# Router logits of the last two pairs from eight more value columns, and two transfers moved behind the value products

## What is computed

```python
def _attn_ref(q, k, v):                      # per batch and head
    scores = scale * np.matmul(q, k.transpose(0, 1, 3, 2))
    kth = np.partition(scores, -top_k, axis=-1)[..., -top_k:-top_k + 1]
    scores = np.where(scores >= kth, scores, -1000000000.0)
    attn = softmax(scores)
    return np.matmul(attn, v)

x = attn_out.transpose(0, 2, 1, 3).reshape(B * S, H * D)   # 1152 x 512
logits = x @ w_gate                          # 512 x 8
expert_idx = np.argmax(logits, axis=1)       # gate_w: its softmax value
# token i takes the next free place (of 288) of its expert, in token order
h = np.maximum(disp[e] @ w1[e], 0.0)         # 512 -> 1024
y = h @ w2[e]                                # 1024 -> 512
out[i] = gate_w[i] * y[expert_idx[i], pos[i]]
```

## Time and profile before

| | us |
|---|---|
| median of 3 runs | 462.11 |
| lowest and highest run | 460.56, 462.35 |
| the profiled execution | 461.55 |
| its span in the trace | 459.8 |

### The profile page before, as it was taken

One profiled execution on the slowest core, in us unless ns is written; L12 is line 12 of the kernel. 1 busy time (PEld: TensorE's weight loads), 2 busy tenths in 40 slices (PEclk: granted clock), 3 DMA queues, 4 the chain that ended last, 5 costly groups with the idle time before them and its releaser, 6 DMA issues.

```text
span 459.8 us, 8667 instructions
## 1 busy us (share of the span) xinstructions
PE 404.1 (88%) x2753; PEld 343.3 (75%) x2753; DVE 288.6 (63%) x1405; ACT 237.8 (52%) x420; POOL 231.7 (50%) x223
## 2 busy tenths in 40 slices
PE   2986768989898898895889998999999999999993
PEld 1553336778686776784779897987999999999771
DVE  2699999899999999989999965401012212121210
ACT  2233358988887887867688992132212121222320
POOL 4044479789888898897799814032001010120310
PEclk9999956999999999999898999999999999999997
DMA  4220132023050230321100105978999685867500
GB/s 103 54 51 3 42 102 52 3 65 107 17 155 1 58 114 1 119 94 70 26 2 2 27 3 163 365 264 259 357 339 339 237 283 185 272 230 247 180 22 19
DMA packets 53633, 57.84 MB, mean 126 GB/s; under 512 B 34382, under 2 KB 34382, under 8 KB 53584
## 3 DMA queue, kind: packets, MB, share of 16 engines
q1 hardware_dynamic: 51408, 52.51, 36.3%
q0 software_dynamic: 2176, 4.73, 2.8%
HBM read 45.39 MB, written 13.92 MB: 129 GB/s over the span
## 4 chain that ended last, share of the span: by engine, by line
PE 35%; POOL 4%; issue 3%; DMA 3%; ACT 2%; DVE 2%; SPq 1%; DVEq 0%; POOLq 0%; ACTq 0%
PE ps_s L865 12%; PE ps_s L883 11%; PE ps_o L665 4%; PE ps_o L840 3%; PE ps_t L637 3%; DMA scores<-dispatched 2%; POOL probs L485 2%; POOL rest L480 1%; ACT pT L972 1%; PE ps_s L691 1%; PE ps_o L821 1%; PE ps_t L809 1%; DMA dispatched<-x,r_slot 1%; ACT probs L954 1%; SPq L405 1%
## 5 line engine op out<-in xcount | busy, mean ns | idle before, releaser
L480 POOL TENSOR_TENSOR rest<-below,scores 128x576 f32<-128x576 f32 x69 | 96.1, 1409 | 47.4 <-DVE below L1137 47.4
L665 PE MATMUL ps_o<-v_aug,pT 128*128 128x128 f32 (+2 forms) x800 | 102.8, 278 | 1.0 <-ACT pT L972 1.0
L665 PEld LDWEIGHTS ps_o<-v_aug,pT 128*128 128x128 f32 (+1 forms) x800 | 96.0, 185 | 2.9 <-issue 1.6
L485 POOL TENSOR_TENSOR probs<-scores,probs 128x576 f32<-128x576 f32 x66 | 93.3, 1431 | 0.7 <-ACT probs L948 0.6
L1072 DVE MAX8 cand<-scores 128x8 f32<-128x96 f32 x432 | 72.7, 257 | 12.1 <-ACT scores L922 12.1
L1038 ACT ACTIVATE scores<-ps_s 128x288 f32<-128x288 f32 x64 | 25.9, 411 | 103.8 <-PE ps_s L865 100.9
L637 PE MATMUL ps_t<-ident,probs 128*128 128x128 f32 (+1 forms) x360 | 55.8, 288 | 21.3 <-ACT pT L972 15.4
L865 PE MATMUL ps_s<-scores 128*128 128x192 f32 (+3 forms) x448 | 66.5, 306 | 0.0
L637 PEld LDWEIGHTS ps_t<-ident,probs 128*128 128x128 f32 (+1 forms) x360 | 38.1, 139 | 36.6 <-issue 21.7
L865 PEld LDWEIGHTS ps_s<-scores 128*128 128x128 f32 x448 | 64.4, 191 | 1.0 <-issue 0.7
L922 ACT ACTIVATE scores<-ps_s 128x576 f32<-128x576 f32 x72 | 46.0, 646 | 36.2 <-PE ps_s L607 20.4
(11 more groups left out here) (138 smaller groups left out, 405.4 us busy)
## 6 DMA issues: line engine op xcount, KB each, us to landing
w_sb<-in_moe_w_dram SPq DMA_DIRECT2D x9, 2048.0 KB, 12.8
scores<-in_moe_w_dram SPq DMA_DIRECT2D x7, 2048.0 KB, 10.9
dispatched<-empty SPq DMA_DIRECT2D x18, 257.0 KB, 3.6
scores<-dispatched SPq DMA_DIRECT2D x21, 192.8 KB
out_dram<-empty SPq DMA_DIRECT2D x9, 256.0 KB, 3.0
q_nat<-in_q_dram SPq DMA_DIRECT2D x16, 128.0 KB, 2.3
k_nat<-in_k_dram SPq DMA_DIRECT2D x16, 128.0 KB, 2.4
v_aug<-in_v_dram SPq DMA_DIRECT2D x16, 128.0 KB, 2.4
```

The costliest lines, as they stand in the source:

```text
L480: nc.gpsimd.tensor_tensor(rest[:, n % 3, :], below[:, n % 3, :], score_tile(n), ALU.mult).then_inc(rest_ready, 1)
L485: nc.gpsimd.tensor_tensor(probs[:, n % PROBS, :], score_tile(n), probs[:, n % PROBS, :], ALU.subtract).then_inc(masked_ready, 1)
L665: last = nc.tensor.matmul(dst, lhs, v_aug[:, g % 2, c, h, 0:width], start=(c == 0), stop=(c == TT - 1))
```

## The change

**Votes instead of logits for pairs 6 and 7.** The product of a head's output with its rows of the gate weights equals the attention applied to (values times gate weights). The change computes that small matrix, 8 columns per head, once per pair and early: SyncE loads the values of pairs 6 and 7 a second time, into the columns of `x` that these pairs will fill later (`values_of`), and the gate weights once more, laid out per head (`wg_heads`). At steps 10 to 13 TensorE transposes them (`turn_values`), ScalarE copies (`copy_vT`), TensorE multiplies (`vote`), and ScalarE keeps the result (`keep_votes`). `place_votes` writes it behind the column of ones in `v_aug` before pair 6 and before pair 7. The value products then give 73 columns per head instead of 65, and `normalise` divides the eight new ones into `voted`. The transposes of `x` for blocks 6 and 7, their copies and their logits are gone. The last head of `x` is scaled (`scale_head`) after the experts of batch 1 are chosen.

**Two transfers later.** SyncE waits for the last value product before it loads the second expert's first weights, and GpSimd waits for it before batch 0's scatter.

The core of the diff:

```diff
-    TURNED = {TILES * 2: 0, TILES * 3: 1, TILES * 4: 2, TILES * 5: 3, TILES * 6 - 2: 4, TILES * 6 + FULL: 5, TILES * 7 + FULL: 6}
-    SPARE = FULL * (D + 1) + P
+    TURNED = {TILES * 2: 0, TILES * 3: 1, TILES * 4: 2, TILES * 5: 3, TILES * 6 - 2: 4, TILES * 6 + FULL: 5}
+    VOTED = PAIRS - 2
+    VOTE_AT = TILES + 1
+    VOTES_AT = {TILES * (VOTED - 1) + 5: 0, TILES * VOTED + 5: 1}
+    WIDE = D + 1 + E
+    SPARE = FULL * WIDE + P
...
+            sp.wait_ge(wg_clean, 1)
+            for h in range(2):
+                sp.dma_start(wg_heads[h * D:(h + 1) * D, :, h, :],
+                             w_gate.rearrange("(c h d) e -> h d c e", h=2, d=D)[h][:, CH - 2:CH]).then_inc(wg_heads_loaded, 16)
+            for i in range(2):
+                load_heads(VOTED + i, v_h, values_of(i).rearrange("p t (h d) -> p t h d", h=2), v_nat_loaded[i])
...
-            sp.wait_ge(masked_ready, 2 * HELD)
+            sp.wait_ge(pv_done, ALL)
             load_w1(1, second)
...
             def scatter_tokens(b):
                 pool.wait_ge(drams_filled, 16 * (E * CAP // P + N // P))
                 pool.wait_ge(slots_ready, b + 1)
+                pool.wait_ge(pv_done, ALL)
+                pool.wait_ge(x_ready, 2 * PAIRS_PER_B * (b + 1))
                 for t in range(TT):
...
             def load_and_transpose(g, transposed):
+                if g == 2:
+                    pe.wait_ge(votes_kept, 4)
 
                 pe.wait_ge(qk_loaded, LOADS * (g + 1))
...
+                    if g >= VOTED:
+                        pe.wait_ge(votes_placed, 2 * (g - VOTED + 1))
...
-                            width = D + 1 if h == 1 and r == FULL - 1 else P
-                            dst = ps_o[:, h, r * (D + 1):r * (D + 1) + width]
+                            width = WIDE if h == 1 and r == FULL - 1 else P
+                            dst = ps_o[:, h, r * WIDE:r * WIDE + width]
...
+            def turn_values(i, naturals):
+
+                pe.wait_ge(v_nat_loaded[i], VLOADS)
+                pe.wait_ge(nat_copied, 2 * naturals)
+                if i > 0:
+                    pe.wait_ge(votes_kept, 2 * i)
+                for t in range(TT):
+                    rows = P if t < FULL else TAIL
+                    last = nc.tensor.transpose(ps_t[:, t * P:t * P + rows], values_of(i)[0:rows, t, :], ident[0:rows, 0:rows])
+                last.then_inc(vT_in_psum, 1)
+
+            def vote(i):
+
+                pe.wait_ge(vT_copied, i + 1)
+                pe.wait_ge(wg_heads_loaded, 32)
+                for t in range(TT):
+                    rows = P if t < FULL else TAIL
+                    last = nc.tensor.matmul(VOTE[0:rows, t * 2 * E:(t + 1) * 2 * E], xT[:, i, t * P:t * P + rows],
+                                            wg_heads[:, i].rearrange("p h e -> p (h e)"), start=True, stop=True)
+                last.then_inc(votes_in_psum, 1)
...
+                if VOTE_AT <= s < VOTE_AT + 4:
+                    if (s - VOTE_AT) % 2 == 0:
+                        turn_values((s - VOTE_AT) // 2, naturals)
+                    else:
+                        vote((s - VOTE_AT) // 2)
...
             pe.wait_ge(hot_placed, TT)
-            place_first_batch(0, 4)
-            transpose_x(2 * CH - 1, ALL)
-            place_first_batch(4, 7)
-            logits(2 * CH - 1)
+            place_first_batch(0, 10)
             carry_ranks()
-            place_first_batch(7, 13)
             router_ranks(1)
-            place_first_batch(13, CH * TT)
+            place_first_batch(10, CH * TT)
+            pe.wait_ge(x_ready, 2 * PAIRS)
...
+            def copy_vT(i):
+                act.wait_ge(vT_in_psum, i + 1)
+                nc.scalar.activation(xT[:, i, 0:S], ps_t[:, 0:S], ACT.Copy).then_inc(vT_copied, 1)
+
+            def keep_votes(i):
+                act.wait_ge(votes_in_psum, i + 1)
+                nc.scalar.activation(votes[:, i, 0:FULL], VOTE[:, 0:FULL * 2 * E].rearrange("p (t h e) -> p t h e", t=FULL, h=2),
+                                     ACT.Copy).then_inc(votes_kept, 1)
+                nc.scalar.activation(votes[0:TAIL, i, FULL], VOTE[0:TAIL, FULL * 2 * E:].rearrange("p (h e) -> p h e", h=2),
+                                     ACT.Copy).then_inc(votes_kept, 1)
+
+            def place_votes(i):
+                g = VOTED + i
+                act.wait_ge(votes_kept, 4)
+                act.wait_ge(pv_done, TILES * (g - 1))
+                nc.scalar.activation(v_aug[:, g % 2, 0:FULL, :, D + 1:WIDE], votes[:, i, 0:FULL], ACT.Copy).then_inc(votes_placed, 1)
+                nc.scalar.activation(v_aug[0:TAIL, g % 2, FULL, :, D + 1:WIDE], votes[0:TAIL, i, FULL],
+                                     ACT.Copy).then_inc(votes_placed, 1)
...
+                if VOTE_AT <= s < VOTE_AT + 4:
+                    if (s - VOTE_AT) % 2 == 0:
+                        copy_vT((s - VOTE_AT) // 2)
+                    else:
+                        keep_votes((s - VOTE_AT) // 2)
+                if p in VOTES_AT:
+                    place_votes(VOTES_AT[p])
...
+                if g >= VOTED:
+                    nc.vector.tensor_tensor(voted[:, n - 2 * VOTED], o_slots[h][:, :, D + 1:WIDE],
+                                            rden[:, h, :].unsqueeze(2).to_broadcast([P, TT, E]),
+                                            ALU.mult).then_inc(voted_ready, 1)
+                if n < 2 * PAIRS - 1:
+                    scale_head(n)
+
+            def scale_head(n):
+
+                g, h = divmod(n, 2)
+                col = (g // PAIRS_PER_B) * PITCH + (g % PAIRS_PER_B) * 2 * D + h * D
                 nc.vector.tensor_tensor(x[:, :, col:col + D], o_slots[h][:, :, 0:D],
                                         rden[:, h, :].unsqueeze(2).to_broadcast([P, TT, D]),
                                         ALU.mult).then_inc(x_ready, 1)
...
             def choose_experts(b):
-                if b == B - 1:
-                    add_logits(PAIRS - 1)
-                dve.wait_ge(log_read, CH * (b + 1))
+                if b == 0:
+                    dve.wait_ge(log_read, CH)
+                else:
+                    dve.wait_ge(voted_ready, 4)
+                    link(nc.vector.tensor_tensor(r_log[:, b], r_log[:, b], voted[:, 3], ALU.add))
                 link(nc.vector.reduce_max(r_max[:, :], r_log[:, b], AX.X))
...
-            dve.wait_ge(logits_done, PAIRS - 1)
+            dve.wait_ge(logits_done, VOTED)
+            dve.wait_ge(voted_ready, 3)
+            linked[0] += 2
             nc.vector.reduce_sum(r_log[:, 1, :, :].rearrange("p t e -> p (t e)"),
-                                 ps_s[:, 0, 0, 0:(CH - 1) * TT * E].rearrange("p (c n) -> p n c", c=CH - 1),
-                                 AX.X).then_inc(log_read, CH - 1)
+                                 ps_s[:, 0, 0, 0:(VOTED - CH) * TT * E].rearrange("p (c n) -> p n c", c=VOTED - CH),
+                                 AX.X).then_inc(route, 1)
+            nc.vector.reduce_sum(r_vote[:, :], voted[:, 0:3].rearrange("p c t e -> p (t e) c"), AX.X).then_inc(route, 1)
+            dve.wait_ge(route, linked[0])
+            link(nc.vector.tensor_tensor(r_log[:, 1, :, :].rearrange("p t e -> p (t e)"),
+                                         r_log[:, 1, :, :].rearrange("p t e -> p (t e)"), r_vote[:, :], ALU.add))
             normalise(PAIRS - 1, 1)
             choose_experts(1)
+            scale_head(2 * PAIRS - 1)
             assign_slots(1)
```

26 lines of the change are left out of this document (21 added, 5 removed).

## The result

| | kernel before | changed kernel |
|---|---|---|
| median of 14 runs each, us | 461.44 (460.18 to 462.94) | 465.62 (462.96 to 468.07) |
| span of the profiled execution, us | 459.8 | 463.9 |

The ratio is 1.0091, with a 95% interval of 1.0074 to 1.0108: slower by 4.2 us. The prediction had 462.6 us and a range that holds 465.6, but its largest chance, 0.48, lay on "same", and "slower" (above 464.4), which came, had 0.30. Its sum was +6.6 early and -5.6 late. The two profiles show +3.3 and +1.0. So one term was too high by 3.3 us and the other too low by 6.6, and that the time still lies in the range is in part luck.

A forecast was written before the change was run, and what follows sets the result against it. VectorE's top-k search was taken to bound the kernel to some 230 us, TensorE from 270 us. From 461.55 us, 6.6 early cost and a 5.6 late gain (6.7 less 1.1) gave 462.6 us, range 458.8 to 466.3.

The forecast's parts named there:

- same: Outcome class for the whole kernel: neither below 459.8 nor above 464.4 us; chance 0.48.
- The early cost: Added vote work after tile 10 delays score tiles and stalls VectorE; 6.6 us lost, bounds nothing to 7.5.
- the first rival: Votes run at TensorE's high clock from 38.7 to 50 us, so the early cost is 4.2; chance 0.17.
- Points 1 and 3 of the late gain: Last pairs' x transposes and logits removed, 1.7 us; shorter chain from values to first expert, 2.5 us.
- point 3: Behind the values: first expert starts 10.45 us after their end instead of 12.92; 2.5 us gained.
- Point 2, the late handoffs: Last tiles' probability copies: two late handoffs vanish as scatters and a load move behind the values; 2.5 us gained.
- the 1.1 us taken off for such things: Deducted from the late gain for handoffs late again and ten scatters beside ranks and first expert; bounds 0 and 2.8.
- Point 4: Ten scatters in a row on GpSimd: the last lands at 301.2, 6.6 us earlier, so next experts' rows do not lag.
- The section on what would show it: Signs to check in the changed timeline: VectorE idle, gate record durations, handoff gaps, 10.5 us to first expert, TensorE waiting for rows.
- The third rival: Late handoffs stay at the last two tiles, or ten scatters disturb ranks and first expert by 2.8; 465.1 us, chance 0.20.

The follow-up runs named there:

- after_rows_first: Changed kernel with the second expert's first weights (2 MB) issued behind the reads of the dispatched rows; 468.13 us, ratio 1.0142.
- after_scatter_early: Changed kernel with batch 0's scatter again starting once its slots are known, the second expert's weights still deferred; 461.72 us, ratio 1.0002.
- after_w1_early: Changed kernel with the second expert's first weights again waiting only for the masked scores, batch 0's scatter still deferred; 466.84 us, ratio 1.0114.
- before_rows_first: Kernel before with only the second expert's first weights moved behind the reads of the dispatched rows; 466.46 us, ratio 1.0125.
- scatter_gap: Changed kernel with batch 1's scatters held until half of batch 1's placement products are done; 466.11 us, ratio 1.0086.
- votes_later: Changed kernel with the turns and votes at steps 16 to 19 in place of 10 to 13; 463.61 us, ratio 1.0048.
- thin_scatter: Changed kernel whose scatters carry 64 of 514 numbers per row into an unread buffer; 457.8 us in one run, not comparable.
- experiment 1: Changed kernel with both, or either, of the two deferrals undone, and kernel before with the deferrals alone; 463.11, 461.72, 466.84 and 460.60 us.
- experiments 2 and 3: Changed kernel with batch 1's scatters held back (465.77, 466.11 us) or thinned (457.8, one run), and with votes at steps 16 to 19 (463.61).
- deferral_only: Kernel before with the two deferrals alone, no votes; 460.60 us, ratio 0.9973.

## Why the prediction came out as it did

*The early cost, 6.6 forecast, 4.5 measured at pair 0, 3.3 at pair 7.* The mechanism was right and the size depends on the clock. With no high clock before 84 us (after_rows_first) the delay at pair 0 is 6.4, the forecast's number. With the high clock from 42 to 49 it is 1.9 and 2.2 (after_scatter_early, after_w1_early), with a short grant at 48 it is 4.4 to 4.9, and with a grant only at 54.6 or 54.8 it is 4.3 and 4.5. So the first rival, at 0.17, named what decides, and got too little weight. Its price was not right: it took 2.4 us off for the whole stretch at the high clock, and that stretch took off 4.2 to 4.5. Its total of 4.2 came near the measured 4.5 with only part of the votes at the high clock. The Trainium skill, page "TensorE: Matmul & The Clock Gate", Part 1, says that activity releases the gate, and had pointed there. What I had not seen at all is the wait for the flag: the text says "nearly no later idle time", and the wait stood in the profile of before. Its 1.3 us are gone in the changed kernel, whose code load falls elsewhere.

*Points 1 and 3 of the late gain held where nothing stalls.* From pair 7 to the first expert's seventh ReLU it takes 25.6 us in the kernel before's order (before_rows_first) and 21.3 in the changed one: 4.3, against 1.7 + 2.5. In the changed kernel's own profile point 3 did not hold: its 10.45 us were 17.2, by the stall.

*Point 2, the late handoffs.* The changed kernel has none, and with scatter 0 undeferred one is back (1.14 us, at 285.18 in after_scatter_early). But before_rows_first has the early scatter and no late handoff. So scatters beside value products are not enough. Point 2 was right for the two profiles compared, not as a rule.

*The failing steps are the 10.45 us of point 3, with the 1.1 us taken off for such things, and point 4.* The first failed in the profile of the changed kernel, by a stall of 6.7 us whose cause is open. The second would have taken the gain without the stall. Point 4 let the last of the ten scatters land 4.09 us behind its start, a duration from a stretch in which the weights had all but arrived (0.3% of the engines), and concluded that the rows "do not lag behind". They landed 8.9 us behind it, and in the other profiles with votes, whole rows and the weights ahead 6 to 8 us behind the last generation. The gain behind the values could not reach the second expert: without a stall, scatter_gap has 45.8 us from pair 7 to the second expert, before 46.2. Of the 7.3 us gained up to the first expert 4.6 go into the wait for rows and most of the rest into the clock. In the changed kernel's own profile the stall took them already: 29.6 + 17.6 = 47.2, +1.0. The section on what would show it named a wait for the third expert's rows; it came one expert sooner, and it belonged into the sum.

*The third rival* named the other half ("if all ten scatters disturb the ranks and the first expert by 2.8"), at about a third of its price: the stall and the slower first expert are 8 us (29.6 against 21.3). In medians the deferral of the scatter costs 3.7 us beside the votes.

*Balance:* +4.5 early, -1.3 at the flag, +1.0 late: 4.2, the distance of the medians; the spans differ by 4.1. The forecast's 1.0 came from +6.6 and -5.6, so its error of 3 us is two larger ones that partly cancel.

**What stays open.** What stalls TensorE in the two profiles with the stall, and what makes handoffs late, is not found. All six profiles that have either were taken on the first two occasions, the eight without them later, where the kernel before itself ran at 459.7 to 460.5 in place of 461.4 to 461.6. Nearly the same program (votes_later, thin_scatter) is among those without. So it may be a condition of the occasion, and not the order; no kernel was profiled in both conditions. That it is the chip is not shown: the runs of experiment 1, which have the stall, and those of experiments 2 and 3, which do not, carry the same chip number, 0. The supply of instructions is a rival that no run tests. In both profiles with the stall a packet of 8 KB of instructions starts 0.2 to 0.4 us after the first gap opens (296.81 against 296.44 in the changed kernel); but scatter_gap has the same packet at 295.99, in the same row of products, and no stall. The 3.7 us that the scatter's deferral costs, and the 1 us that deferral_only gains, hold for the first condition alone. No version was faster than the kernel before by more than that.

## What to carry to other kernels

When a change shortens the compute chain, add up the bytes that must be through before the next step's data can land, from the first issue of that stretch: here the rows came 26 us behind the lead's weights, with 1.6 us of slack, and that was the bound to check. A landing time read in a stretch with empty queues does not hold in a full one, and a load that is moved behind another also meets what is queued after it. If a wait is left in TensorE's way, arriving earlier at it may cost clock. And where a delay seems to be paid back at a later wait, look at that wait in a run without the delay: here it was gone there too.

## What was not expected of the hardware

- In two profiles TensorE took placement records singly, one each 0.72 us, for 5 to 7 us, with no semaphore to wait for; it began 7.6 us behind the first of ten scatter generations and ended 1 to 2 us behind the last.
- TensorE was granted 2.4 GHz at quite different times by kernels that are the same up to there: at 42.3, 42.5, 48.1, 48.8, 48.9, 54.6 and 54.8 us, and once not before 84.5. One term of 2 to 6.4 us hangs on it, and the changed kernel's runs spread over 5 us where before's spread over 2.8.
- A wait of 2.7 to 4.8 us in front of a long row of products came with another 1.7 to 3 us and a fall to 1.2 GHz (in votes_later from 308.4 to 315.2 us).
- A DMA of 0.5 KB took 3.2 us in place of 1.9 with a packet of 16 KB of instructions beside it (before, at 201.56 us). Of 149 such flags in 14 profiles all eight that took more than 2.6 us had one.
